# A fused attention, gated and convolved mixer on one core: low parts of two weight matrices made by TensorE, softmax parts placed singly, new orders at both ends

## The reference

```python
# stage 1: 7-tap mix of tokens, weights from a softmax over the taps
w = softmax(weight_gen, axis=-1)                       # (2, 4160, 8 heads, 7 taps)
a[b, s, h, :] = sum_k w[b, s, h, k] * x_pad[b, s + k, h, :]
# stage 2: d_model 192, d_ff 1024
xk = mu_k * a + (1 - mu_k) * a_prev                    # a_prev: one token earlier
xr = mu_r * a + (1 - mu_r) * a_prev
y  = sigmoid(xr @ w_r) * (maximum(xk @ w_k, 0) ** 2 @ w_v)
# stage 3
h  = maximum(y @ w_in, 0)
c  = sum_k conv_w[k] * h_pad[:, k:k + S, :]            # 3 taps along the tokens
out = (h * sigmoid(c)) @ w_out
```

## Time and profile before

| | us |
|---|---|
| median of 3 runs | 723.04 (722.88 to 723.24) |
| the profiled execution's own time | 723.3 |
| its span | 721.5 |
| PE busy | 703.1 (97%) |
| DVE busy | 673.5 (93%) |
| ACT busy | 630.2 (87%) |

### The profile page before, as it was taken

The page is one execution under the profiler, slowest core; times in us unless marked ns, Lnnn a source line. Parts: engine busy times, 40 slices in busy tenths (PEclk is TensorE's granted clock), DMA queues, the critical chain, the costliest instruction groups (busy, mean ns, idle before and its releaser), DMA issues.

```text
span 721.5 us, 10642 instructions
## 1 busy us (share of the span) xinstructions
PE 703.1 (97%) x3556; PEld 601.9 (83%) x3556; DVE 673.5 (93%) x991; ACT 630.2 (87%) x1272; POOL 3.6 (0%) x12
## 2 busy tenths in 40 slices
PE   5889999999999999999999999999999999999997
PEld 5777778888888888888888888888888888888997
DVE  7998999989999999989999999989999899887788
ACT  3789797979999797989999798989979798998986
POOL 1000000000000000000000000000000000000000
PEclk9999999999999999999999999999999999999999
DMA  5711010100202010010201001020101002000000
GB/s 143 252 56 55 1 55 1 56 22 1 78 0 78 1 55 22 16 63 0 77 1 56 22 9 70 1 77 1 55 23 56 22 1 73 0 23 1 23 14 36
DMA packets 9067, 28.81 MB, mean 40 GB/s; under 512 B 1310, under 2 KB 3896, under 8 KB 8886
## 3 DMA queue, kind: packets, MB, share of 16 engines
q1 hardware_dynamic: 8856, 28.12, 11.6%
q10 hardware_dynamic: 158, 0.03, 0.0%
HBM read 21.75 MB, written 6.39 MB: 39 GB/s over the span
## 4 chain that ended last, share of the span: by engine, by line
PE 82%; DVE 10%; issue 3%; ACT 2%; DMA 1%; SPq 1%; DVEq 0%; ACTq 0%
PE up L337 36%; PE od L442 22%; PE dn L404 4%; PE dn L420 4%; PE dn L423 4%; PE dn L424 4%; PE dn L427 4%; PE dn L426 3%; DVE att L1715 2%; DVE prod L1703 2%; PE mid L308 2%; DVE kq_lo L1779 1%; DMA h<-in_moe_w_k 1%; DVE cv L1827 1%; DVE cv L1814 1%
## 5 line engine op out<-in xcount | busy, mean ns | idle before, releaser
L442 PE MATMUL od<-wo_sb,gat 128*128 128x192 f32 x1040 | 182.2, 326 | 1.6 <-ACT o_sb L929 1.0
L442 PEld LDWEIGHTS od<-wo_sb,gat 128*128 128x128 f32 x1040 | 172.7, 190 | 8.6 <-DVE gat L1836 1.3
L1779 DVE TENSOR_TENSOR kq_lo<-ksq,kq_hi 128x512 fp32r<-128x512 f32 (+2 forms) x136 | 89.7, 661 | 17.6 <-ACT kq_hi L875 17.3
L1814 DVE SCALAR_TENSOR_TENSOR cv<-h,prm,cv 128x512 f32<-128x512 f32 (+1 forms) x136 | 96.8, 723 | 5.4 <-ACT cv L911 4.4
L1827 DVE SCALAR_TENSOR_TENSOR cv<-h,prm,cv 128x512 f32<-128x512 f32 (+1 forms) x136 | 97.9, 721 | 0.1
L911 ACT ACTIVATE cv<-h,prm 128x512 f32<-128x512 f32 (+1 forms) x136 | 94.1, 695 | 1.9 <-DVE gat L1836 1.4
L900 ACT ACTIVATE h<-up 128x512 f32<-128x512 f32 (+2 forms) x136 | 77.8, 573 | 19.6 <-PE up L337 17.2
L1715 DVE TENSOR_TENSOR att<-att,prod 128x768 f32<-128x768 f32 (+1 forms) x102 | 94.6, 927 | 0.4
L1703 DVE TENSOR_TENSOR prod<-xin,wgt 128x768 f32<-128x768 f32 (+1 forms) x102 | 93.3, 928 | 0.5
L1836 DVE TENSOR_TENSOR gat<-h,cv 128x512 f32<-128x512 f32 (+1 forms) x136 | 88.4, 661 | 1.5 <-ACT cv L918 1.2
L859 ACT ACTIVATE ksq<-up 128x512 f32<-128x512 f32 (+2 forms) x136 | 78.3, 576 | 11.3 <-PE up L337 9.1
(11 more groups left out here) (110 smaller groups left out, 1334.0 us busy)
## 6 DMA issues: line engine op xcount, KB each, us to landing
xin<-in_x SPq DMA_DIRECT2D x14, 960.0 KB, 4.7
out<-o_sb SPq DMA_DIRECT2D x16, 384.0 KB, 2.3
wgt<-in_weight_gen SPq DMA_DIRECT2D x1, 1092.0 KB, 11.0
xin<-in_x SPq DMA_DIRECT2D x1, 864.0 KB, 4.7
h<-in_moe_w_v SPq DMA_DIRECT2D x1, 768.0 KB, 4.8
wo_sb<-in_moe_w_out SPq DMA_DIRECT2D x1, 768.0 KB, 12.4
h<-in_moe_w_k SPq DMA_DIRECT2D x1, 512.0 KB, 5.3
h<-in_moe_w_k SPq DMA_DIRECT2D x2, 256.0 KB, 6.5
```

What stands on the lines that cost most here:

```text
L442: mm = nc.tensor.matmul(o, tile[:, b * P:(b + 1) * P], wo_sb[:, c, :], start=(c == 0 and b % 2 == 0), stop=(c == NC - 1), skip_group_check ...
L1779: nc.vector.tensor_tensor(ring(kq_lo, c, n), ring(ksq, c, n), ring(kq_hi, c, n).bitcast(F32), ALU.subtract).then_inc(kql_ok, 1)
L1814: nc.vector.scalar_tensor_tensor(o, win(w, c, -1), prm[:, 3 + c:4 + c], o, ALU.mult, ALU.add)\
```

## The change

Four things change. The low parts of w_k and w_v no longer come from DVE: for each piece PE adds the raw float32 weight times the identity and the high part times minus the identity in one PSUM bank, and ACT copies the sum to its place (`low_wk` and `keep_wk`, 4 pieces of 512 columns; `low_wv` and `keep_wv`, 4 pieces of 384). In the first two steps SP issues w_k ahead of `prm_rows`, and w_r is issued by ACT, with no wait for w_k. The softmax parts of groups 3, 7 and 11 are called singly at chosen places. And all three order lists are written anew, with fewer warm transposes (103 instead of 173), `r_part(g, 1)` within `up2(g - 1)`, and `down2` of a window spread later.

```diff
@@ sync
             for a, b in HALO_RUNS:
                 sp.dma_start(xin[a:b, 0:TAPS * D], before(x_flat, a, b, TAPS, D)).then_inc(x_in, 16)
+            load_up_weights(sp, w_k, 0, wk_in)
             for r, src in enumerate((mu_k, mu_r)):
...
-            load_up_weights(sp, w_k, 0, wk_in)
-
-            sp.wait_ge(wk_in, 48)
-            for c0, c1, at in ((0, D, 0), (P, D, D)):
-                sp.dma_start(raw_wr[:, 0, at:at + c1 - c0], w_r[0:P, c0:c1]).then_inc(wr_in, 16)
...
@@ tensor
+            def low_part(o, raw, hi, arrived, split, count, done):
+
+                rows = raw.shape[0]
+                pe.wait_ge(*arrived)
+                nc.tensor.matmul(o, ident[0:rows, 0:rows], raw, start=True, stop=False)
+                pe.wait_ge(minus_ok, 1)
+                pe.wait_ge(split, count)
+                nc.tensor.matmul(o, minus[0:rows, 0:rows], hi, start=False, stop=True).then_inc(done, 1)
...
             def first_steps():
+                low_wk(0)
+                low_wk(1)
+                low_wk(2)
+                warm(6)
+                low_wv(0)
                 t_part(0, 1)
                 t_part(0, 2)
-                warm(23)
+                low_wk(3)
+                low_wv(1)
+                warm(3)
                 up1(0, 0)
                 up1(0, 1)
...
@@ scalar
+                    load_wr()
+                    nc.scalar.activation(minus[:, :], ident[:, :], ACT.Copy, scale=-1.0).then_inc(minus_ok, 1)
...
+            def keep_wk(k):
+                cols = slice(k // 2 * BANK, (k // 2 + 1) * BANK)
+                act.wait_ge(lowk_done, k + 1)
+                nc.scalar.activation((wk_lo, wk2_lo)[k % 2][:, cols], (up[0], up[1], dn[0], dn[1])[k][:, :], ACT.Copy)\
+                    .then_inc(w_split, 1)
...
                 cast_wk()
                 cast_wr()
+                keep_wk(0)
+                cast_wv()
+                keep_wk(1)
                 double(0)
+                keep_wv(0)
                 z_part(0, 0)
...
@@ vector
-            def split_wv():
-                dve.wait_ge(wv_cast, 2)
...
```

More of the change, by code:

```diff
@@ L536, in first_steps @@
                 down2(1, 3)
-            def step(i):
-                down2(i - 2, 4)
+                up2(2, 0)
+                up2(2, 1)
+                up2(2, 2)
+                down2(1, 4)
+                up2(2, 3)
+                up2(2, 4)
+                up2(2, 5)
+                r_part(3, 1)
+                up2(2, 6)
+                up2(2, 7)
+                up1(3, 0)
+            def step(i):
+                up1(i - 1, 1)
+                up1(i - 1, 2)
+                r_part(i - 1, 2)
+                up1(i - 1, 3)
+                down2(i - 3, 5)
+                up1(i - 1, 4)
+                down1(i - 1, 0)
+                down1(i - 1, 1)
+                up1(i - 1, 5)
+                down1(i - 1, 2)
+                up1(i - 1, 6)
+                down2(i - 3, 6)
+                down1(i - 1, 3)
+                up1(i - 1, 7)
+                t_part(i, 1)
+                down1(i - 1, 4)
+                down2(i - 3, 7)
+                t_part(i, 2)
+                down1(i - 1, 5)
+                down1(i - 1, 6)
+                down1(i - 1, 7)
+                down2(i - 2, 0)
+                down2(i - 2, 1)
+                down2(i - 2, 2)
+                down2(i - 2, 3)
                 up2(i - 1, 0)
@@ L546, in step @@
                 up2(i - 1, 5)
-                down2(i - 2, 6)
+                r_part(i, 1)
                 up2(i - 1, 6)
@@ L584, in last_steps @@
                 up2(NG - 6, 5)
-                down2(NG - 7, 6)
+                r_part(NG - 5, 1)
                 up2(NG - 6, 6)
@@ new lines, in first_steps @@
+                gate_sigmoid(3, 4)
+                carry(3, 1)
+                y_hi_part(4, 1)
+                carry(3, 2)
+                y_hi_part(4, 2)
+                gate_sigmoid(3, 5)
+                y_hi_part(4, 3)
+                x_hi(5, 1)
+                carry(3, 3)
+                carry(3, 4)
+                h_relu(4, 0)
+                first_tap(4, 0)
+                h_relu(4, 1)
+                xr_hi_part(5, 2)
+                h_relu(4, 2)
+                gate_sigmoid(3, 6)
@@ L1662, in _ @@
             first_steps()
-            for i in range(3, NG - 5):
+            for i in range(4, NG - 5):
                 step(i)
```

1494 lines of the change are left out of this document (815 added, 679 removed).

## The result

The changed kernel takes 725.64 us in the median of 6 runs (724.73 to 726.38), the kernel before 723.09 (722.88 to 723.24): ratio 1.0035, 95% interval 1.0026 to 1.0045. It is slower, where the prediction said 721.5 and a gain.

A forecast was written before the change was run, and what follows sets the result against it. PE was taken to bound 80 to 693 us except one gap, with DVE saturated in parts of head and tail. Head -0.2, middle -0.5 and tail -0.8 sum to -1.5 on 723.04: 721.5 us, range 718.2 to 724.5 for 8 in 10.

The forecast's parts named there:

- T: Head: the first transpose of the mix, `t_part(0, 1)`, forecast at 22.7 us.
- When PE starts: Head: parameters land about with w_k, so PE starts at 12.5 us; bounds 8.36 and 13.2.
- The price of the f32 product: Head, low parts on PE: 0.85 ns a column, 0.44 us for 512 columns; a w_k piece 0.67, a w_v piece 0.50.
- the rival that held it: Head: f32 products cost twice the forecast price, 1.65 us more ahead of the transposes, 723.1 us; chance 0.03.
- Warming products: Head: 40 warm transposes on PE, 21 at 0.21 us and 19 at 0.109, take 6.5 us.
- The credits of 0.87 and 1.83: Head, DVE: `att_mult(1, 0)` behind `mix_k(0)` (0.87) and no `split_wv` (1.83) offset `mix_k(0)` running 2.8 us late.
- -1.16 + 1.2 - 0.75: Head, later: `r_part(1, 1)` within `up2(0)` -1.16; table load before `h_relu(0, 7)` +1.2; the old load's wait gone -0.75 us.
- 4.2 off DVE: Head: `split_wk` (2.33 us) and `split_wv` (1.83) leave saturated DVE; alone, `up2(0, 0)` would start 4.2 us earlier.
- Middle: PE's 0.53 us gap between 400 and 402 us vanishes with softmax parts set apart: -0.5 us; bounds 0 and -0.53.
- Tail: One `down2` chunk instead of two before `up2(NG-1, 0)` ends its first chunk earlier: gain 0.8 us, bounds 0 and -1.3.
- Early parameters: Rival, head: parameters land early, PE starts at 8.4 us and `mix_k(0)` runs 3.1 us sooner, 718.4 us; chance 0.20.
- ACT as the bound: Rival, head: ACT's added copies and recurring waits make `y_hi_part` 3.1 us late, 724.6 us; chance 0.17.

The follow-up runs named there:

- e1: Changed kernel with the five small parameter loads issued ahead of w_k's three on SP's queue again: 721.65 us.
- e4: Changed kernel with the f32 product in each low part of w_k and w_v replaced by a second fp32r product (wrong low parts): 724.04 us.
- e6: e1 with `r_sigmoid(1, 1)` moved behind `h_relu(0, 7)` on ACT: 721.08 us.
- e13: e9 with the low parts of w_k and w_v made by DVE again and warming products in place of PE's low parts: 722.88 us.
- e9: e1 with 24 instead of 40 warming products at the start and `r_sigmoid(1, 1)` behind `h_relu(0, 7)`: 719.12 us.
- e10: e9 with DVE's `softmax_back(7)` moved from ahead of `k_lo(4, 5)` to behind `k_lo(4, 7)`: 723.53 us.
- e12: e9 with DVE's `conv_after(3, 4)` moved behind `k_lo(4, 5)`: 719.50 us.
- e7: e1 with the tail's old order, `down2(NG - 2, 5)` ahead of `up2(NG - 1, 0)`, put back: 721.62 us.
- e8: e1 with DVE's `att_mult(1, 0)` moved behind `mix_k(0)`, `mix_r(0)` and `mix_2(0)`: 722.23 us.
- e5: e1 with 24 instead of 40 warming products at the start: 720.11 us.
- e11: e10 with 12 instead of 24 warming products at the start: 723.06 us.

## Why the prediction was wrong

The profiled spans differ by +3.0 us, the prediction's sum was -1.5: 4.5 us to account for. They lie at T 2.6 (25.34 against 22.7 forecast), from T to W 0.4 (54.52 against 76.99 - 0.2 - 22.7 = 54.09), in the middle 1.1, in the tail 0.35.

- **When PE starts.** The mechanism was right and put first: "this decides most". The parameters landed behind w_k, at 13.5 instead of 12.5 and 0.3 beyond the upper bound, 13.2; PE started 1.1 us later than forecast. w_k landed for 12.86, no sooner than before, as forecast. By the Trainium skill, DMA: Bandwidth & Descriptors, section Queues, rings and completion order, the descriptors of one ring are taken in order; the 6.81 us of the 12 KB of `conv_w` behind w_k, against 8.36 - 4.62 = 3.74 ahead of it, agree. e1 shows that this order alone cost 4.0 us of median. The measured time turns on this start, and its size, put 1.1 us too small, is the first of the two terms that failed ahead of T.
- **The price of the f32 product.** The step "a plain f32 product of 192 columns costs 5.20 / 32 = 0.163 us" failed. The trace keeps two matmul records for each f32 product: `x2` stands at L332 for one product in the code, and e4, which replaces 8 such products by fp32r ones, has 3502 matmuls where the changed kernel has 3510. So the earlier trace rows show 16 products in 5.20 us, 0.325 each, 1.69 ns a column, and the measured 0.86 / 512 is 1.68. The page FP8 and Floating Point Precision of the Trainium skill, section TensorE Precision Notes, was right with its four passes: the estimate worked out from them was 1.1 for the piece, the measured piece is 1.09 (20.75 to 21.84). I read the trace as speaking against it, because I divided by records and not by products: the `x8` of two `down2` chunks in the order of instructions above is `x16` in the earlier trace rows. On T this is 3 x 0.42 + 0.33 = 1.6 us. That e4 also gave 1.6 us of median is chance: it takes away nearly the whole product and not only what was missing in its price. Its 2.2 us against the 0.8 by the forecast prices bear out 1.4. This is the second term that failed; the rival that held it had a chance of only 0.03, since "the rows are of the same kind of product", which they are, at twice the price.
- **Warming products.** Forecast 6.5 for the 40, 6.84 in the chain: 0.3, which the 0.3 that the sum had between the last product and the transposes makes up for.
- **After T.** Only 0.4 off in the sum, but partly by luck, since two parts were off in opposite directions. From T to the last product of `up2(0, 0)` the forecast was 48.5 - 22.7 = 25.8, and 25.5 were measured (25.34 to 50.84; before 19.48 to 47.97, so 28.49). All of the gain of 3 us lies here. The credits of 0.87 and 1.83 were rightly placed: `att_mult(1, 0)` stands behind the mix before and ahead of it after, where it writes over the source of the transposes and so waits for T. From there to W the forecast was -1.16 + 1.2 - 0.75 = -0.7, and nothing was gained (29.02 before and after). The table load costs 0.6 (e6) and not 1.2, so the two gains of 1.16 and 0.75 together gave 0.6 and not 1.9; which of them failed was not tested.
- **What the change is for.** "4.2 off DVE" was right: e13 gives 3.8 us of median. It was hidden by the late T: 7.1 us of DVE idle stand where the 4.2 us of work had been.
- **Middle.** W to D is 0.6 longer instead of 0.5 shorter. The step that failed is "set apart by three steps it should vanish": the softmax parts still fall on DVE's full list, now at two places. The rows of before (first) and after:

```profile
400.55 0.50 PE L420 MATMUL dn<-kq_hi,wv_parts 128*128 128x512 f32 x1 [0.54 <-DVE kq_lo L1779]
...
193.37 0.50 PE L440 MATMUL dn<-kq_hi,wv_parts 128*128 128x512 f32 x1 [0.34 <-DVE kq_lo L1946]
...
400.68 0.60 PE L305 MATMUL mid<-ident,att 128*128 128x128 f32 x4
401.38 0.50 PE L440 MATMUL dn<-kq_hi,wv_parts 128*128 128x512 f32 x1
```

  The wait at 400 us hides in the last two: only 0.1 us of idle time shows, but the runs of 32 `down2` products around it start 83.51 us apart (321.76 and 405.27), where two periods are 83.0, so 0.5 is lost; in e9 the chain leads there from a softmax part through `k_lo` to PE. At 193.37, where `softmax_back(7)` stands ahead of `k_lo(4, 5)`, the period is 42.22 instead of 41.5, so 0.7. Before, the one wait made two periods 83.84, so 0.86. The two now less the one then are 0.4 of the 0.6; the rest was not followed. Neither e10 nor e12 gained anything.
- **Tail.** -0.46 measured, -0.8 forecast; the reason given for it is refuted by e7, which undoes the move in e1 and loses at most 0.1. The first `up2` chunk does end 0.5 sooner after `down1` (2.8 us instead of 3.3; forecast 2.55), but nothing behind it needed that. What makes the 0.46 was not tested.
- **The rivals.** Early parameters, 718.4: e1 is that kernel and took 721.65, because T still came 2.1 us after the sum was ready: PE started at 9.04, and the f32 products cost more than was forecast. e9, in which T meets the sum as that rival had it, took 719.12. ACT as the bound gave 724.6, the nearest number, by the wrong mechanism: ACT was busy 7.24 of 10 from 20 to 30 us and waited 6.1 us for PE's first low part.

## What to carry to other kernels

An engine taken off the critical path gives its time only if nothing else arrives later: before crediting it, work out the arrival of every input of the next step, here one transpose that waited for five small loads behind 1 MB of weights. Put small loads that start an engine ahead of large ones on the same queue, and count warming products as work once the chain runs through them (24 instead of 40, parameters first and one table load moved: 719.12 us instead of 725.64). Take the price of an operation from products in the code, not from records in the trace; a count that doesn't match the loop is a warning. In a full list, moving one piece moves the wait (e10, e12).

## What the runs showed of the hardware

- **The slow start of TensorE varies.** The 40 warming products took 6.57 (e1), 6.74 (e7), 6.91 (changed), 6.98 (e6) and 7.49 us (e8), and 6.11 in e4. At 0.22 us for a slow product (e5) and 0.109 for a fast one that is an estimated 3.5 to 6 us at half pace, the 1.2 GHz level by spacing, while the granted clock reads 1.00 there.
- **Where it counts, runs differ more.** Where PE's own chain sets T, the runs of a kernel spread over 1.65 us (changed, 6 runs), 1.6 (e1, 11) and 2.2 (e8, 11). Where T waits for the sum of the mix, PE's slow start is covered: before 0.57 (29 runs), e13 0.50 (11). The start of PE with the parameters first also varied, 8.77 to 10.02, where w_r's loads from ACT's queue run beside them. That the spread has these two causes was not tested by itself. e9, in which T just meets the sum, spread over 1.48 (5 runs), one of them 1.1 above the rest; e10 and e11 spread wider, 3.2 and 2.7, with their loss in the middle.
- **A short wait can cost twice, or once.** In e10, 2.0 us of PE waits were followed by ten microseconds at a granted clock of 0.83; the loss was 4.1 us. In e11, which has the same waits, it was 3.8 (W to D 618.35 against 614.57), with a granted clock of 0.95 and 0.88 in the windows from 190 and from 200 us, so 1.7 us again. In e5 the granted clock gave up the same 1.7 us in the head, and the time from T to W did not change, because VectorE was the limit there. In these runs a lower clock cost time only where TensorE was the limit.
